# A recurrence and two gated layers on one core: one load overtakes another, the weights' low parts come a round later, round 11 is reordered, and the first r is shared out differently

## The reference

```
state = 0                                            # per batch and head, 48 x 48
for t in range(768):                                 # r, k, v, w: (2, 8, 768, 48); u: (8, 48)
    y[t]  = r[t] @ (state + outer(u * k[t], v[t]))
    state = w[t][:, None] * state + outer(k[t], v[t])
x = y as (2, 768, 384)
h = gelu(x @ w_in); u, v = halves of h               # w_in: 384 x 1024
v = (v - mean) / sqrt(var + 1e-6) * g_ln
x = x + (u * (w_sg @ v + b_sg)) @ w_out              # w_sg: 768 x 768
x = x + (relu(x^T @ tok1) @ tok2)^T                  # 768 -> 256 -> 768
x = x + relu(x @ ch1) @ ch2                          # 384 -> 1536 -> 384
```

## Time and profile before

| what | value |
|---|---|
| median of 3 runs | 368.2 us |
| the profiled execution's own time | 369.53 us |
| its span, first to last instruction | 368.0 us |
| TensorE busy | 359.9 us, 98% |
| GpSimd busy | 188.6 us, 51% |
| VectorE busy | 163.0 us, 44% |
| ScalarE busy | 106.6 us, 29% |
| chain that ended last | PE 84%, POOL 8%, issue 3%, DVE 3%, ACT 1% |
| DMA | 29.78 MB, mean 81 GB/s |

### The profile page before, as it was taken

How to read it: one execution, slowest core, us unless ns; L and a number is a source line. 1 busy time by engine, 2 the same in 40 slices (tenths; PEclk the granted TensorE clock), 3 DMA queues, 4 the chain that set the end, 5 groups by cost and what they waited for, 6 DMA issues and landing times.

```text
span 368.0 us, 6598 instructions
## 1 busy us (share of the span) xinstructions
PE 359.9 (98%) x2620; PEld 322.8 (88%) x2620; DVE 163.0 (44%) x272; ACT 106.6 (29%) x205; POOL 188.6 (51%) x191
## 2 busy tenths in 40 slices
PE   8999898999999999999999999999999999999996
PEld 8788787998999999999999998888888888888885
DVE  7989886656203323583469443340033300233100
ACT  3876267546450044310121312330022200132000
POOL 5997999999684465779999940037000000000000
PEclk9999999999999999999999999999999999999999
DMA  7985993311122000021223400000000000000011
GB/s 239 412 289 183 369 381 114 109 45 45 43 90 83 3 1 0 2 86 45 86 87 128 128 2 0 2 2 28 30 28 0 2 28 28 30 0 0 2 47 38
DMA packets 12463, 29.78 MB, mean 81 GB/s; under 512 B 1680, under 2 KB 5904, under 8 KB 12432
## 3 DMA queue, kind: packets, MB, share of 16 engines
q1 hardware_dynamic: 12432, 29.35, 22.8%
HBM read 26.99 MB, written 2.36 MB: 80 GB/s over the span
## 4 chain that ended last, share of the span: by engine, by line
PE 84%; POOL 8%; issue 3%; DVE 3%; ACT 1%; DVEq 0%; POOLq 0%
PE bank L1269 25%; PE bank L1268 25%; PE bank L1270 25%; PE bank L1291 2%; PE bank L1355 2%; PE bank L1454 2%; POOL sg_lo L621 1%; PE bank L1400 1%; POOL rp L677 1%; POOL rku L640 1%; POOL yt L693 1%; POOL rku L632 1%; POOL rstd L703 1%; PE bank L1301 1%; PE bank L1333 1%
## 5 line engine op out<-in xcount | busy, mean ns | idle before, releaser
L902 ACT ACTIVATE ha_hi<-bank 128x512 fp32r<-128x512 f32 x36 | 21.6, 601 | 106.6 <-PE bank L1270 106.6
L1176 DVE SCALAR_TENSOR_TENSOR ha_lo<-bank,ha_hi 128x512 fp32r<-128x512 f32 x36 | 24.9, 692 | 50.6 <-ACT ha_hi L902 50.6
L1268 PE MATMUL bank<-ha_hi,c_lo 128*128 128x512 f32 x108 | 42.1, 390 | 0.0
L1270 PE MATMUL bank<-u2T_hi,c_hi 128*128 128x512 f32 x108 | 42.0, 389 | 0.0
L1269 PE MATMUL bank<-u2T_lo,c_hi 128*128 128x512 f32 x108 | 42.0, 389 | 0.0
L1270 PE MATMUL bank<-ha_hi,c_hi 128*128 128x512 f32 x108 | 42.0, 389 | 0.0
L1269 PE MATMUL bank<-ha_lo,c_hi 128*128 128x512 f32 x108 | 42.0, 389 | 0.0
L1268 PE MATMUL bank<-u2T_hi,c_lo 128*128 128x512 f32 x108 | 42.0, 389 | 0.0
L1268 PE MATMUL bank<-sg_hi,z_lo 128*128 128x384 f32 x96 | 32.1, 334 | 0.0
L1269 PE MATMUL bank<-sg_lo,z_hi 128*128 128x384 f32 x96 | 32.1, 334 | 0.0
L1270 PE MATMUL bank<-sg_hi,z_hi 128*128 128x384 f32 x96 | 32.1, 334 | 0.0
(11 more groups left out here) (144 smaller groups left out, 833.6 us busy)
## 6 DMA issues: line engine op xcount, KB each, us to landing
turned<-in_turned_all SPq DMA_DIRECT2D x9, 772.0 KB, 7.7
raw<-in_moe_w_ch SPq DMA_DIRECT2D x12, 384.0 KB, 3.1
rows<-in_rows_all SPq DMA_DIRECT2D x6, 576.0 KB, 7.0
raw<-in_moe_w_sg SPq DMA_DIRECT2D x6, 384.0 KB, 3.0
out<-x2T SPq DMA_DIRECT2D x8, 256.0 KB, 2.0
raw<-in_moe_w_in SPq DMA_DIRECT2D x4, 384.0 KB, 5.0
raw<-in_moe_w_tok SPq DMA_DIRECT2D x4, 384.0 KB, 3.2
rows<-in_rows_all SPq DMA_DIRECT2D x6, 192.0 KB, 5.5
```

The lines of the kernel that those rows point to most:

```text
L902: sc.activation(ha[0][:, i, :], bank[:, :], ACT.Relu).then_inc(act_out, 1)
L1176: ve.scalar_tensor_tensor(ha[1][:, i, :], bank[:, :], 0.0, ha[0][:, i, :].bitcast(F32), ALU.max, ALU.subtract).then_inc(dve_out, 1)
L1268: te.matmul(dst, left[1], right[0], start=first, stop=False)
L1270: return te.matmul(dst, left[0], right[0], start=False, stop=last)
```

## The change

It has four parts.

1. SP issues the rows of chunk 6 ahead of weight piece 2 (w_in 0), not behind it.
2. GpSimd's low parts come a round later: w_in 1 in round 8 (was 7), w_sg 0 in round 9 (was 8), w_sg 1 in round 10 (was 9), w_sg 2 after round 11 together with w_sg 3 to 5 (was round 10). w_in 0 stays in round 6. On ScalarE the high part of w_in 0 moves from the end of round 5 to round 6, behind the xT job and ahead of `take_state`; w_in 1 stays at the end of round 6.
3. In round 11 GpSimd makes yt ahead of the reciprocal deviation of v tile 5, and ScalarE normalizes that tile after the six xT jobs of batch 1, not before the first of them.
4. In chunk 0 VectorE scales three pairs of r (128x384 is 3 pairs of 128) and GpSimd one. TensorE takes the pairs in the order 1, 2, 3, 0. VectorE's part also waits for its own first scan, `pre0_half`.

```diff
@@ load order on SP
             load_raw(1)
+            load_rows(6)
             load_raw(2)
-            load_rows(6)
             load_turned(7)
@@ GpSimd, first r
-                gp.tensor_tensor(rp[0:QP, 0, 0:2, :], kr_tile(0, 1)[:, 0:2, :], pre_tile()[:, 0:2, :], ALU.mult
+                gp.tensor_tensor(rp[0:QP, 0, 0:1, :], kr_tile(0, 1)[:, 0:1, :], pre_tile()[:, 0:1, :], ALU.mult
@@ GpSimd, rounds 6 to 11
-            low = {6: [("w_in", 0)], 7: [("w_in", 1)], 8: [("w_sg", 0)], 9: [("w_sg", 1)], 10: [("w_sg", 2)]}
+            low = {6: [("w_in", 0)], 8: [("w_in", 1)], 9: [("w_sg", 0)], 10: [("w_sg", 1)]}
...
-                if len(last) == 1:
+                early = len(last) == 1 and n < NCH - 1
+                if early:
                     rstd_tile(*last[0])
...
                 diagonal_v(n)
-                if len(last) > 1:
+                if not early:
...
-                for i in range(3, NC):
+                for i in range(2, NC):
                     split_low("w_sg", i)
@@ ScalarE
-            high = {5: [("w_in", 0)], 6: [("w_in", 1)], 7: [("w_sg", 0)], 8: [("w_sg", 1)],
+            high = {7: [("w_sg", 0)], 8: [("w_sg", 1)],
...
                     take_job(*job)
+                if n == YR + 1:
+                    split_high("w_in", 0)
                 if n % NC < NC - 1:
                     take_state(n)
                 for job in slot_jobs(n, 2):
                     take_job(*job)
-                for piece in high[n]:
-                    split_high(*piece)
+            split_high("w_in", 1)
...
-                if len(last) == 1:
+                if len(last) == 1 and n < NCH - 1:
                     normal(*last[0])
...
+                if (kind, b, i) == ("xT", 1, NC - 1):
+                    normal(*v_jobs(NCH - 2)[0])
@@ VectorE, first r
                 wait_r(dve, 0)
+                dve.wait_ge(pre0_half, 1)
                 dve.wait_ge(pre_done, 1)
-                ve.tensor_tensor(rp[0:QP, 0, 2:NP, :], kr_tile(0, 1)[:, 2:NP, :], pre_tile()[:, 2:NP, :], ALU.mult
+                ve.tensor_tensor(rp[0:QP, 0, 1:NP, :], kr_tile(0, 1)[:, 1:NP, :], pre_tile()[:, 1:NP, :], ALU.mult
@@ TensorE, scores
-                for p in (range(NP) if n else (2, 3, 0, 1)):
+                for p in (range(NP) if n else (1, 2, 3, 0)):
```

## The result

The changed kernel takes 366.85 us (median of 6 runs, 366.52 to 367.25) against 368.58 for the kernel before measured beside it (6 runs, 368.17 to 369.44). The ratio is 0.9951, 95% interval 0.9938 to 0.9963: some 1.8 us faster, where 2.5 were forecast. The profiled executions differ by more: the span fell from 368.0 to 365.0 us, by 3.0. That the traces show 3.0 and the medians 1.8 is what the experiments had to explain.

What follows compares the result with a forecast made beforehand. TensorE was taken as the bound, busy 359.9 of 368.0 us, with 2.78 us of waits in reach. Terms 0.89 + 1.15 + 0.1 + 0.41 - 0.05 = 2.50, from 368.2 to 365.7 us; range 365.0 to 367.1.

Steps and rivals of the forecast that it cites:

- Rival A: Chunk 6's rows come no earlier, or something else held it; 0.89 goes, 1.61 us gained, 366.6 us; chance 0.15.
- B: Rival: GpSimd stays the bound into round 9, part 3 hidden by yt's wait; gain 1.5, 366.7 us; chance 0.12.
- Part 1, the rows, 0.89: Chunk 6: rows issued one issue earlier end TensorE's 1.22 us wait before new_part; 0.89 us kept.
- Part 2, the low parts, 1.15: Chunk 9: without w_in_lo in front, GpSimd's rp(9) ends earlier and TensorE's wait before the scores goes; gain 1.15 us.
- 0.1 for small waits: Rounds 7 and 8: v and u products wait less for ScalarE to empty a bank; 0 to 0.2, taken 0.1 us.
- The slack called on: Rows of chunks 10 and 11, held behind loads awaiting low parts, still land in time; chunk 10 slack over 3 us.
- Part 3, 0.41: Round 11: earlier xT copies end TensorE's wait before batch 1's first v job; gain 0.41 us, bounds 0 and 0.41.
- Part 4, 0.05 lost: Chunk 0: VectorE's third pair ends its part 0.13 us later; loss 0.05, bounds gain 0.1 and loss 0.24.
- Rival C: Round 7: weight piece 2 lands late and holds ScalarE's take_state and v tile; slower, 368.9 us; chance 0.03.

Runs made afterwards that it cites:

- low parts alone: Kernel before with only GpSimd's low parts a round later; ScalarE's order, rows, round 11 and first r as before: 366.87 us, ratio 0.9954.
- part 2 alone: Kernel before with low parts a round later and ScalarE's high part of w_in 0 moved: 367.46 us, measured again 367.13.
- low parts undone: Changed kernel with GpSimd's low parts back at their earlier rounds, ScalarE's order still changed: 368.10 us, ratio 0.9971.
- first group's kernel before: Kernel before, unedited, measured beside the kernels that each undo one part of the change: 369.08 us (17 runs).
- part 1 undone: Changed kernel with the rows of chunk 6 loaded behind weight piece 2 again: 366.81 us, ratio 0.9941.
- part 3 undone: Changed kernel with round 11 as before, on GpSimd and on ScalarE: 366.70 us, ratio 0.9936.
- rows later still: Changed kernel with chunk 6's rows loaded behind weight piece 2 and chunk 7's transposed inputs: 369.48 us, ratio 1.0019.
- parts 1 and 2: Changed kernel with round 11 and the sharing of the first r put back as before: 366.93 us, ratio 0.9946.
- part 4 undone: Changed kernel with the first r shared two pairs and two between VectorE and GpSimd as before: 366.95 us, ratio 0.9939.

## Why the prediction was right, and where it was off

**The range held and the mechanisms were those foreseen, but the forecast of 365.7 was 1.15 low and its own band, 365.2 to 366.3, was missed.** The measured time lies in the range only because rivals A and B widened it. By the steps, each with what the two traces show and what the medians do:

- *Part 1, the rows, 0.89.* The mechanism is as told: the rows were what chunk 6 waited for, and passing one load removes the wait: none of the five traces with it waits, six of the eight without it do. In the two traces it is worth even more, 1.18 by chunk 8. But the term was mis-sized for the median: it was read from one execution whose rows took 7.0 us to land, the longest of eight traces. Undone, it cost nothing measurable (366.81 against 366.85); the low parts alone, without it, are as fast (366.87); beside part 2 alone it was worth 0.2. This is the step that failed.
- *Part 2, the low parts, 1.15 and 0.1 for small waits.* Right: rp(9) predicted for 59.66 was at 59.72, the distance from chunk 8's scores to chunk 9's fell by 1.23 (10.30 to 9.07), and undoing it costs 1.25 (368.10 against 366.85). The small waits are there, 0.23, but the table shows that they go with the wait for the rows and not with the low parts: 52.66 - 44.93 = 7.73 from chunk 7 to 8 with the low parts undone, as short as in the changed kernel. The slack called on held: GpSimd took the rows of chunks 10 and 11, now behind loads that wait for these low parts, at 71.69 and 79.97 without a wait, and the product with w_sg moved up by the full 3.00.
- *Part 3, 0.41.* The wait goes, but the credit was given to the wrong part. On the kernel before it is worth 0.76 by itself, in the changed one 0: GpSimd, early by part 2, already removes the wait. The low parts alone reach 366.87 without it. In the sum this does no harm, as the wait was counted once. Its size was read too small: TensorE's transposes need 1.94 us until the next product can start (84.11 to 86.05), not the 2.19 of the modelled row that the prediction subtracted, so the wait in the earlier trace rows was 0.66 (2.60 - 1.94).
- *Part 4, 0.05 lost.* VectorE's row of three pairs took 0.71 us at 6.22, and the first scores started at 7.08 instead of 6.90. The prediction took the row's length for the engine's own work; part of it is waiting for GpSimd (hardware section). Nothing of it is left at 36 us: the scores of chunk 6 are at 36.11 against 36.07, and undoing it changed nothing.
- *Rival C*, weight piece 2 late for ScalarE: piece 2 landed at 32.21 + 6.0 = 38.2, long before ScalarE used it at 40.88. No trace shows it.

The traced sizes are 1.18, 1.23, 0.66 and a loss of 0.04: 3.03, the 3.0 between the two spans. Without part 1 they are 1.85, and the medians differ by 1.73, with an interval of 1.4 to 2.3. So the typical execution of the kernel before seems to have lost next to nothing to the rows. This is inferred, since only the traced executions show the wait itself; and against the first group's kernel before the gain would be larger, up to 2.4. Rivals A (1.61 gained) and B (1.5) came closer to the measured gain than the forecast's 2.5, but not for their reasons: in the trace the rows were earlier and nothing else held chunk 6, and GpSimd did not stay the bound. Rival A's number fits because the same 0.89 drops out of the sum.

Why two traces differ by 3.0 us: the profiled execution of before, 369.53, lies 0.95 above its median, and that of after, 366.52, 0.33 below; 3.0 - 0.95 - 0.33 = 1.7. How much of the 0.95 is the long wait for the rows and how much the ordinary spread no run separates: the first scores alone start anywhere from 6.84 to 7.49 in these traces. A like number was on the page when the prediction was made, the 1.3 us between the profiled execution and the 368.2 of the runs; it was treated as an offset that both kernels share, when part of it may have been the very wait that the change removes.

What stays open: why a built program tends to land the rows early or late. Low parts alone and part 1 undone had no wait and runs within 1 us, part 2 alone had one in both of its traces, though SP's list is the same in all four. The long issue on SP and the landing go together in some traces (issues of 1.7 to 1.8 us for the two pieces come with the waits, 0.81 and 1.43 with none), which may be the cause or a sign of it; no experiment changed it.

No version beats the changed kernel beyond its interval. The low parts alone (366.87) and part 3 undone (366.70) are equal to it with less change; the order of the rows is worth keeping as a guard, since every trace with it is free of the wait.

## What to carry to other kernels

A wait for a DMA in one trace is one draw from a spread (5.9 to 7.0 us to land for the same load, in eight traces): before pricing its removal, take a second and third trace, and give the term a range that starts at nothing. The distance of the profiled execution from the median of the runs is a hint at most: it was 0.95 above with the longest wait, but part 2 alone lost 0.62 to the rows in an execution 0.17 under its median. When several waits lie one behind another on the same late engine, price them together: making the engine early in one place (a low part moved behind the operand that TensorE waits for) removed two waits, and the edit that aimed at the second won nothing beside it. And let a moved instruction's slack be read off the timeline of the engine that will wait, load by load; here that gave GpSimd's starts to within 0.1 us (rp(8) at 50.56 against 50.54, rp(9) at 59.72 against 59.66).

## What the runs showed of the hardware

**Behind a long wait of TensorE the granted clock fell.** In the kernel with the rows later still, TensorE's granted clock falls to half (the 1.2 GHz level) just after its wait of 1.66 us. The windows of TensorE alone: length, its busy time, granted clock, DMA share, GB/s.

```profile
39.00:40.00 1.00, 0.00 (x0) 1.00 1.01 418
40.00:41.00 1.00, 0.69 (x15) 0.70 1.00 374
41.00:42.00 1.00, 1.00 (x24) 0.50 1.01 355
42.00:43.00 1.00, 1.00 (x21) 0.50 1.02 409
43.00:44.00 1.00, 1.00 (x6) 0.59 1.01 395
44.00:45.00 1.00, 1.00 (x6) 1.00 0.97 378
```

The same `new_part` takes 1.90 us there instead of 1.14:

```profile
40.31 1.90 PE L1360 MATMUL bank<-rows,am 128*64 128x48 f32 x32 [1.66 <-issue]
```

Half of this kernel's twelve runs had a mean clock of 0.995 or less, and they took 369.8 to 372.1 us, the others 367.5 to 369.2. Of the 58 runs of the kernel before beside the experiments five had such a clock, and they took 369.5 to 370.3; of the changed kernel's six runs none had. A fall is not tied to that long wait: in the trace of parts 1 and 2 (368.30, its other runs 366.64 to 367.10) the clock fell at 19 to 23 us, some 2 us after a wait of 0.59 before the scores of chunk 2. All fourteen traces have that wait, 0.33 to 0.60 us long (0.56 in the kernel before, 0.59 in the changed one), and in the other thirteen the clock stayed:

```profile
17.04 1.59 PE L1292 MATMUL bank<-rp,kp 48*128 48x128 f32 x16 [0.59 <-issue]
...
19.93 1.53 PE L1346 MATMUL bank<-sbd,rp 112*64 112x96 f32 x16
...
23.57 0.60 PE L1292 MATMUL bank<-rp,kp 48*128 48x128 f32 x6
```

```profile
19.00:20.00 1.00, 1.00 (x22) 0.95 0.68 232
20.00:21.00 1.00, 1.00 (x16) 0.50 0.45 112
21.00:22.00 1.00, 1.00 (x25) 0.50 0.52 153
22.00:23.00 1.00, 1.00 (x26) 0.50 0.90 369
23.00:24.00 1.00, 1.00 (x22) 0.84 0.70 290
```

The next scores start at 23.57, 6.53 us after those of chunk 2, where the other thirteen traces have 4.85 to 5.13. Waits of 1.22 and 1.15 us in the kernel before went without a loss of clock in its trace. So a fall came behind a wait in some executions and not in others with the same wait; what decides it no run here shows. Here a long wait carried a risk for the clock beside its own length: six of twelve runs with the rows later still, against five of 58 of the kernel before; at which point the untraced runs lost their clock is not recorded.

**VectorE and GpSimd took turns at the first r.** The length of a row here is not the work of its engine. GpSimd's kp of chunk 0, then the two parts of the first r, in the changed kernel:

```profile
5.33 1.18 POOL L661 TENSOR_TENSOR kp<-turned,suf 112x512 f32<-112x512 f32 x1 [2.92 <-DMA turned<-in_turned_all]
...
6.22 0.71 DVE L1084 TENSOR_TENSOR rp<-turned,pre 112x384 f32<-112x384 f32 x1
6.48 0.72 POOL L668 TENSOR_TENSOR rp<-turned,pre 112x128 f32<-112x128 f32 x1
```

and GpSimd's kp in the kernel before, whose two parts are in the earlier trace rows:

```profile
5.25 1.19 POOL L661 TENSOR_TENSOR kp<-turned,suf 112x512 f32<-112x512 f32 x1 [2.83 <-DMA turned<-in_turned_all]
```

VectorE's row starts while kp still runs and ends 0.42 after it (6.93 against 6.51) with three pairs, 0.28 after it (6.72 against 6.44) with two; GpSimd's part ends 0.27 after VectorE's (7.20) with one pair and 0.54 after it (7.26) with two. Twelve of the fourteen traces have these numbers within 0.02 us, though VectorE's row is 0.43 to 0.85 us long for two pairs and 0.56 to 0.98 for three. In the other two GpSimd's part began first, and the order is turned. In that of parts 1 and 2, where kp ended at 6.13 and VectorE started at 6.14, VectorE's two pairs end 0.28 after GpSimd's two (7.05 against 6.77):

```profile
6.09 0.68 POOL L668 TENSOR_TENSOR rp<-turned,pre 112x256 f32<-112x256 f32 x1
6.14 0.91 DVE L1080 TENSOR_TENSOR rp<-turned,pre 112x256 f32<-112x256 f32 x1
```

In that of the low parts undone kp ended at 6.00, GpSimd's single pair was done at 6.37, and VectorE's three pairs took 0.56 from 6.23, near the 0.547 of the shortest 384-wide row. So each engine's row contains the time until the other's ended. A pair costs VectorE 0.14 and GpSimd 0.27 once it has its turn; the third pair on VectorE is 0.14 us later for TensorE, and much of the rest of the spread of the first scores comes from when GpSimd's kp ends (6.00 to 6.96). With part 4 undone kp ended at 6.96, VectorE's part at 7.24, and the first scores began at 7.40. Spans on GpSimd are rough, but the differences agree over the traces.

This agrees with what the Trainium skill says of such a pair of instructions (SBUF - State Buffer, "SBUF: two separate sides"), the sentence that the prediction weighed: the one that starts first has the shared ports for the whole instruction.
